# Sparse attention with two MLP layers: the context of 384 queries in one visit instead of two

## The reference

```python
scores = scale * np.matmul(q, k.transpose(0, 1, 3, 2))
thresh = np.max(scores, axis=-1, keepdims=True) - tau
scores = np.where(scores >= thresh, scores, -1e9)
scores = scores - np.max(scores, axis=-1, keepdims=True)
attn = np.exp(scores)
attn = attn / (np.sum(attn, axis=-1, keepdims=True) + 1e-9)
x = np.matmul(attn, v)                    # then to (2304, 512)
h = np.maximum(x @ w_in, 0.0)             # (2304, 2048)
x = (s * h * h + b) @ w_out               # first layer, (2304, 512)
h = x @ w_in2
y = (h / (1.0 + np.exp(-1.702 * h))) @ w_out2
```

## Time and profile before

| | us |
|---|---|
| median of 3 runs | 1021.88 |
| lowest, highest | 1020.71, 1023.87 |
| the profiled execution | 1022.94 |
| its span, first to last instruction | 1021.1 |
| PE busy | 989.9 |
| DVE busy | 801.5 |
| POOL busy | 657.9 |
| ACT busy | 605.1 |

### The profile page before, as it was taken

How to read it: one execution, slowest core, us unless ns; L and a number is a source line. 1 busy time by engine, 2 the same in 40 slices (tenths; PEclk the granted TensorE clock), 3 DMA queues, 4 the chain that set the end, 5 groups by cost and what they waited for, 6 DMA issues and landing times.

```text
span 1021.1 us, 18040 instructions
## 1 busy us (share of the span) xinstructions
PE 989.9 (97%) x5832; PEld 890.1 (87%) x5832; DVE 801.5 (78%) x1755; ACT 605.1 (59%) x1112; POOL 657.9 (64%) x714
## 2 busy tenths in 40 slices
PE   5978999999999999999999999999999999999998
PEld 4867888888888888888899999898988989889897
DVE  5999999999999999999646766877667777556563
ACT  5876665666676667665545755654546545454453
POOL 5758997778888788887657775444544544445442
PEclk9999999999999999999999999999999999999999
DMA  6228777688877887768733540112123121231212
GB/s 194 89 77 228 219 203 221 173 242 226 211 208 186 236 209 214 206 177 215 205 122 125 184 148 32 39 66 83 42 83 123 63 83 43 82 132 55 83 47 78
DMA packets 101420, 144.26 MB, mean 141 GB/s; under 512 B 10704, under 2 KB 72784, under 8 KB 101328
## 3 DMA queue, kind: packets, MB, share of 16 engines
q1 hardware_dynamic: 101328, 143.11, 48.5%
HBM read 102.96 MB, written 4.72 MB: 105 GB/s over the span
## 4 chain that ended last, share of the span: by engine, by line
PE 82%; DVE 12%; issue 2%; DMA 2%; ACT 1%; POOL 1%; SPq 0%; DVEq 0%; ACTq 0%; POOLq 0%
PE shared L810 12%; PE y_ps L829 11%; PE y_ps L927 9%; PE shared L903 9%; PE scores L927 9%; PE scores L729 7%; PE scores L903 7%; PE scores L786 6%; PE scores L810 5%; PE y_ps L849 4%; DVE scores L1010 4%; DVE prob L1036 3%; DVE blocks L1050 2%; PE scores L849 1%; DMA a_raw<-twin_in 1%
## 5 line engine op out<-in xcount | busy, mean ns | idle before, releaser
L1229 ACT ACTIVATE prob<-scores,neg_max 128x576 f32<-128x576 f32 (+1 forms) x160 | 118.9, 743 | 132.2 <-DVE scores L1010 130.0
L1568 POOL TENSOR_TENSOR a_sum_lo<-a_sum,a_hi 128x256 fp32r<-128x256 f32 x96 | 70.0, 740 | 187.4 <-DVE scores L1132 124.6
L1517 POOL TENSOR_TENSOR w_lo<-w_raw,win_hi 128x512 fp32r<-128x512 f32 x96 | 129.0, 1344 | 23.0 <-ACT win_hi L1267 18.7
L1010 DVE TENSOR_SCALAR_CACHE_REDUCE scores<-scores,consts 128x576 f32<-128x576 f32 (+1 forms) x160 | 129.3, 808 | 16.3 <-PE scores L729 14.8
L1524 POOL TENSOR_TENSOR w_lo<-w_raw,wout_hi 128x512 fp32r<-128x512 f32 x96 | 125.7, 1310 | 23.2 <-ACT wout_hi L1274 23.2
L1511 POOL TENSOR_SCALAR prob<-prob,row_inv 128x576 f32<-128x576 f32 (+1 forms) x160 | 126.1, 800 | 12.0 <-DVE row_inv L1024 11.7
L1036 DVE SCALAR_TENSOR_TENSOR prob<-scores,limit,prob 128x576 f32<-128x576 f32 (+1 forms) x160 | 128.3, 809 | 0.8 <-DVE limit L1017 0.5
L810 PE MATMUL shared<-act_hi,win_hi 128*128 128x384 f32 x280 | 95.3, 340 | 5.4 <-DVE gate L1066 3.4
L1050 DVE STREAM_TRANSPOSE blocks<-prob 128x576 f32<-128x576 f32 (+1 forms) x136 | 97.2, 752 | 3.1 <-DMA prob_t<-blocks 2.8
L810 PE MATMUL shared<-act_hi,w_lo 128*128 128x384 f32 x280 | 95.0, 339 | 0.0
L810 PE MATMUL shared<-act_lo,win_hi 128*128 128x384 f32 x280 | 94.5, 338 | 0.0
(11 more groups left out here) (154 smaller groups left out, 2934.3 us busy)
## 6 DMA issues: line engine op xcount, KB each, us to landing
w_raw<-slabs SPq DMA_DIRECT2D x93, 512.0 KB, 4.2
a_raw<-twin_in SPq DMA_DIRECT2D x24, 512.0 KB, 4.6
o_raw<-twin_out SPq DMA_DIRECT2D x24, 512.0 KB, 3.6
prob_t<-blocks SPq DMA_DIRECT2D x96, 120.0 KB, 2.8
k_raw<-k SPq DMA_DIRECT2D x32, 288.0 KB, 4.5
prob_t<-blocks SPq DMA_DIRECT2D x96, 96.0 KB, 2.8
v_sb<-v SPq DMA_DIRECT2D x26, 320.0 KB, 4.3
q_raw<-q SPq DMA_DIRECT2D x40, 192.0 KB, 4.5
```

Of the source, the lines that this page charges most:

```text
L1010: nc.vector.tensor_scalar(place, place, scale_c[0:m, :], None, ALU.mult, ALU.min, accum_out=neg_max[0:m, j % STATS:j % STATS + 1]).then_in ...
L1229: nc.scalar.activation(prob[0:m, j % PROBS, :].rearrange("p (a n) -> p a n", a=2), scores[j % 2][0:m, :, 0:HALF], ACT.Exp, bias=neg_max[0: ...
L1517: nc.gpsimd.tensor_tensor(in_of(w_lo, n), in_of(w_raw, n), win_hi[n % IN_HI][:].bitcast(F32), ALU.subtract).then_inc(win_lo_ready, 1)
```

## The change

The two pieces of a long group become one of 384 queries. It rides on one beat, 7 behind the group's first (6 for w = 29, which HASTY now names as well as w = 11): 10 matmuls into columns 288 to 479 of the first bank of the second tile's buffer, a wait for quads 2 and 3, and 10 matmuls into the same columns of the second bank. ScalarE and VectorE each take 384 columns in one instruction. The moves into either half of `prob_t` now wait for the whole piece of a long group, and a short group behind a long one has all three quads in the beat four behind its first. Long groups from w = 12 on are 12, so 40 riding pieces become 28. Short groups keep their pieces' places.

```diff
-HASTY = 3 * PAIRS_PER_BATCH - 1
+HASTY = (3 * PAIRS_PER_BATCH - 1, len(GROUPS_OF) - 3)
...
-        after = 3 if w < PE_GROUPS else 5 if w == HASTY else 6
-        pieces += [(w, n, FIRST_BEAT[w] + after + n) for n in range(3 if w < PE_GROUPS else 2 if is_long(w) else 1)]
+        if w < PE_GROUPS:
+            pieces += [(w, n, FIRST_BEAT[w] + 3 + n) for n in range(TILES_PER_HEAD[LONG])]
+        else:
+            pieces.append((w, 0, FIRST_BEAT[w] + (7 if is_long(w) else 6) - (1 if w in HASTY else 0)))
...
-    return PIECE if rides(piece) else P
+    return GROUPS_OF[PIECES[piece][0]][3] if rides(piece) else P
...
-                   if n < w and (n % 2 == 0 if n < PE_GROUPS else (place if is_long(n) else half_of(n)) == half))
+                   if n < w and (n % 2 == 0 if n < PE_GROUPS else is_long(n) or half_of(n) == half))
...
-            return scores[1][:, 1, HALF:HALF + PIECE] if rides(piece) else shared[:, 0:P]
+            if not rides(piece):
+                return shared[:, 0:P]
+            return scores[1][:, 0 if is_long(PIECES[piece][0]) else 1:2, HALF:HALF + SHORT]
...
-                    if beat == FIRST_BEAT[w] + (4 if is_long(w) else 3) + a // 2:
+                    if beat == FIRST_BEAT[w] + (4 + a // 2 if is_long(w) else 4 if is_long(w - 1) else 3 + a // 2):
                         move_quad(w, a)
...
+                for n in range(piece_size(piece) // SHORT):
+                    quads = (2 * n, 2 * n + 1) if is_long(w) else (0, 1, 2)
+                    for a in quads:
+                        half = moved_into(w, a)
+                        pe.wait_ge(moved[half][a], 64 * moves_before(w + 1, half, a))
+                    start = LONG * (n if is_long(w) else half_of(w))
+                    for c in range(KEY_CHUNKS):
+                        for side in range(2):
+                            place = piece_bank(piece)[64 * side:64 * side + 64, n, :]
...
+                            mm = nc.tensor.matmul(place.rearrange("p (a q) -> p a q", a=len(quads)),
+                                                  v_sb[:, i % 2, side, c, :], rows,
+                                                  start=(c == 0), stop=(c == KEY_CHUNKS - 1))
                 mm.then_inc(context_ready, 1)
...
-                nc.vector.tensor_tensor(act_at(act_lo, c, start, piece_size(piece)), piece_bank(piece),
-                                        act_at(act_hi, c, start, piece_size(piece)).bitcast(F32),
+                nc.vector.tensor_tensor(piece_of(act_lo, piece), piece_bank(piece), piece_of(act_hi, piece).bitcast(F32),
...
-                nc.scalar.copy(act_at(act_hi, c, start, piece_size(piece)), piece_bank(piece)
-                               ).then_inc(context_hi_ready, 1)
+                nc.scalar.copy(piece_of(act_hi, piece), piece_bank(piece)).then_inc(context_hi_ready, 1)
```

More of the change, by code:

```diff
@@ L34 @@
 LONG, SHORT = 384, 192
-PIECE = SHORT
 TILES_PER_HEAD = {LONG: 3, SHORT: 2}
@@ L290, in pieces_on @@
 def pieces_on(w, half):
-    return 1 + max(piece for piece, (n, place, _) in enumerate(PIECES)
-                   if n < w and (n % 2 == 0 if n < PE_GROUPS else (place if is_long(n) else half_of(n)) == half))
+    return 1 + max(piece for piece, (n, _, _) in enumerate(PIECES)
+                   if n < w and (n % 2 == 0 if n < PE_GROUPS else is_long(n) or half_of(n) == half))
 def value_loads():
@@ L595, in piece_bank, with piece_of @@
         def piece_bank(piece):
-            return scores[1][:, 1, HALF:HALF + PIECE] if rides(piece) else shared[:, 0:P]
+            if not rides(piece):
+                return shared[:, 0:P]
+            return scores[1][:, 0 if is_long(PIECES[piece][0]) else 1:2, HALF:HALF + SHORT]
+        def piece_of(parts, piece):
+            c, start = piece_place(piece)
+            place = act_at(parts, c, start, piece_size(piece))
+            return place.rearrange("p (n q) -> p n q", q=SHORT) if rides(piece) else place
         block = ctx.enter_context(nc.Block())
@@ L761, in context_of @@
                 w, n, _ = PIECES[piece]
[L762 to L767, removed]
+                i = VALUE_OF[piece]
+                pe.wait_ge(v_loaded[i % 2], 16 * (i // 2 + 1))
+                if not rides(piece):
                     pe.wait_ge(tail_copied, FIRST_BEAT[w] + n + 1)
@@ L772, in context_of @@
                         pe.wait_ge(context_lo_ready, piece)
[L773 to L779, removed]
+                    for c in range(KEY_CHUNKS):
+                        for side in range(2):
+                            start = LONG * side + P * n
+                            mm = nc.tensor.matmul(piece_bank(piece)[64 * side:64 * side + 64, :],
+                                                  v_sb[:, i % 2, side, c, :], turned_rows(w)[:, c, start:start + P],
+                                                  start=(c == 0), stop=(c == KEY_CHUNKS - 1))
@@ new lines, in context_of @@
+                    mm.then_inc(context_ready, 1)
+                    return
+                for n in range(piece_size(piece) // SHORT):
[4 more added lines that the diff above has]
+                    start = LONG * (n if is_long(w) else half_of(w))
+                    for c in range(KEY_CHUNKS):
+                        for side in range(2):
+                            place = piece_bank(piece)[64 * side:64 * side + 64, n, :]
@@ L1054, in context_lo @@
             def context_lo(piece):
-                c, start = piece_place(piece)
                 dve.wait_ge(context_hi_ready, piece + 1)
-                nc.vector.tensor_tensor(act_at(act_lo, c, start, piece_size(piece)), piece_bank(piece),
-                                        act_at(act_hi, c, start, piece_size(piece)).bitcast(F32),
+                nc.vector.tensor_tensor(piece_of(act_lo, piece), piece_bank(piece), piece_of(act_hi, piece).bitcast(F32),
                                         ALU.subtract).then_inc(context_lo_ready, 1)
@@ L1233, in context_hi @@
             def context_hi(piece):
-                c, start = piece_place(piece)
                 act_eng.wait_ge(context_ready, piece + 1)
-                if start >= HALF_TOKENS and piece_place(piece - 1)[1] < HALF_TOKENS:
+                if piece_place(piece)[1] >= HALF_TOKENS and piece_place(piece - 1)[1] < HALF_TOKENS:
                     act_eng.wait_ge(scores_ready, key_tiles(2 * HEADS_PER_BATCH - 1)[-1] + 1)
-                nc.scalar.copy(act_at(act_hi, c, start, piece_size(piece)), piece_bank(piece)
-                               ).then_inc(context_hi_ready, 1)
+                nc.scalar.copy(piece_of(act_hi, piece), piece_bank(piece)).then_inc(context_hi_ready, 1)
             def copy_main(j):
```

## The result

| us | before | after |
|---|---|---|
| median, beside each other, 6 runs each | 1022.31 | 1027.76 |
| lowest, highest | 1020.71, 1023.87 | 1026.94, 1029.59 |
| the profiled execution | 1022.94 | 1027.94 |
| its span | 1021.1 | 1026.2 |

The ratio is 1.0057 (95%: 1.0046 to 1.0068): slower by 5.5 us, more than the 0.3% that can be told from no change. The forecast was 1027.1 us.

What follows compares the result with a forecast made beforehand. TensorE and VectorE were both taken as nearly full, the order of light and heavy beats deciding which waits. +2.9 and +2.4 made +5.3 us on the profiled 1022.94, 1028.2; as median 1027.1, range 1019.5 to 1033.5.

Steps and rivals of the forecast that it cites:

- The order of beats, +2.9: Beats 31 to 77: two beats without a visit in a row cost VectorE more than TensorE needs; +2.9 us, bounds -2.0 and +5.
- The single spans: Visit start to visit start: 24.3 us over three N (beats without a visit), 20.14 per three-beat period, 32.6 per five-beat period.
- The 0.77 us of a beat with context: VectorE's wait for the second tile's scores before row_max in a beat with a visit, time it cannot save up.
- The moves of w = 29, +2.4: Beat 79: quads 2 and 3 land late, TensorE stops 2.1 us mid-visit (bounds 0 and 5); +2.4 us in all.
- the moves elsewhere, costed at nothing: Other groups' moves start later but stay hidden, in long groups but for half a microsecond at worst; no cost.
- rival 4: Transfers late everywhere: each of eleven long groups behind a double visit loses 0.5 us; 1033 us, chance 0.12.
- The visit itself: A double visit takes TensorE 2 x 1.77 = 3.54 us; 12 changes of 0.17 us fall away, 2.0 us off TensorE.
- VectorE's idle time ahead of the second row_max: Sign: in each double-visit beat this idle time grows to over 2 us.
- The idle times in front of double visits: Sign: TensorE waits 0.3 to 0.8 us for VectorE's mask in front of each double visit.
- Rival 1: Fewer, wider instructions win: 1018.3 us, chance 0.07; test: beat 38's visit starts under 15.9 us after beat 35's ends.

Runs made afterwards that it cites:

- e3: The changed kernel with all four quads' 16 moves of a long group in one row, ahead of the loads between: 1024.96 us, 1.0027 of the kernel before.
- the light row_max: row_max on the first 288 keys alone, in three kernels: before 1012.81 us, after 1013.38, after with the 16 moves in one row 1009.11.
- e1: The changed kernel, but w = 29 keeps its two visits in beats 79 and 80: 1025.62 us, 1.0030 of the kernel before.
- e2: The kernel before with the double visit for w = 29 alone: 1023.20 us, 1.0012 of the kernel before.
- g2: e3 with row_max on the first 288 keys alone: 1009.11 us, 0.9866 of the kernel before.
- b: The kernel before with row_max on the first 288 keys alone: 1012.81 us, 0.9916 of the kernel before.
- e4: The kernel before, its visits and moves kept, but 384-column copies behind a long group's second visit (not w = 29): 1023.36 us, 1.0012 of before.
- f2: e3 with gated_lo ahead of the second row_max in every beat with a visit: 1024.67 us, 1.0031 of the kernel before.
- f1: The kernel before with gated_lo ahead of the second row_max in every beat with a visit: 1024.11 us, 1.0022 of the kernel before.
- g1: e3 with gated_lo ahead of the second row_max in double-visit beats alone: 1023.05 us, 1.0004 of the kernel before.
- g4: g1 with the first tile's mask also ahead of the second row_max in double-visit beats: 1024.63 us, 1.0022 of the kernel before.
- a: The changed kernel with row_max on the first 288 keys alone: 1013.38 us, 0.9923 of the kernel before.

## Why the prediction was right

- **The order of beats, +2.9.** Right, and shown by itself in e3: 301.33 us from beat 31 to 77 against 301.3, without a late move. That VectorE causes it is shown by the light row_max: without late moves in front of the double visits merging costs 2.6 us with the full one and gains 3.1 with the light one. The single spans in e3 came out near what was worked out: 24.3 for three N, 19.8 to 20.7 for periods of three beats (20.14 forecast), 32.6 to 32.9 for those of five (32.6). That the sum agrees to 0.1 us is in part chance: the visits were 0.14 us shorter than in the forecast and the spans between them about as much longer. The 0.77 us of a beat with context was read from one beat; before, such waits were 0.2 to 0.8 us long.
- **The moves of w = 29, +2.4.** The gap was 2.44 us against 2.1. From beat 77's visit to beat 84's it is 43.97 us against 39.83, 4.14 longer; the forecast's share was 2.4 and 1.77 for the longer last visit, 4.17. By e1 the shares were 2.5 and 1.63. Its cause was told too simply: in e2, where the group before is not merged, the gap is 0.83 us. That nothing behind it takes the time back was said from the earlier trace rows, which end at 494.64; it held, with 507.6 us from beat 84's visit to the end of the span before and 507.8 after.
- **The term that was mis-sized: the moves elsewhere, costed at nothing.** "Hidden too, but for half a microsecond at worst" held for the gap (0.54 us in beat 38, and a smaller one in beat 57), not for what follows: from 31 to 77 the kernel after took 302.69 us against e3's 301.33, so 1.4 us, a part of rival 4. In it are the two gaps and the waits of transposes for `blocks`, 3.8 us of VectorE's time after and none in e3, which were not tried apart. I had taken its bound from one landing of 5.8 us; after, landings of 6.8 and 7.6 us stood behind four loads.
- **What made up for it.** By these spans the kernel should be 2.51 + 4.14 = 6.65 us slower. Beat 31's visit came 1.78 us earlier in the profiled execution, for which see the last section, and so the profiled executions are 5.0 us apart where the forecast had 5.3. That is luck. How much of it is in the medians, which lie 5.5 us apart, is not known, since the starts of the other runs are not; their interval, 4.7 to 7.0 us, holds both the forecast and the 6.65.
- **The visit itself.** Forecast 3.54 us, measured 3.40: for the twelve, 1.7 us less of TensorE's time than I had. That the changes to and fro fell away shows in g2 against b, where TensorE decides; in the kernel after nothing of either is gained.
- **Not as foretold.** VectorE's idle time ahead of the second row_max did not grow to over 2 us in each double visit: up to beat 77 it was 0.4 to 2.1 us and in one of them nothing, with 1.3 to 1.4 the usual, and only in beat 79, with its stop, 4.2. A VectorE that comes late has less to wait. The idle times in front of double visits were 0.16 to 0.67 us where 0.3 to 0.8 stood; a part of the lateness shows at `hidden`, which waits for `gated` (1.3 us in seven waits).

Rival 1's test, the visit of beat 38 within 15.9 us of the end of that of 35, fails: 216.09 - (196.06 + 3.40) = 16.63. The rule behind it (the Trainium skill, Perfetto Trace Analysis, Optimizing Scalar/DVE Operations) on wider operations is borne out in their total and not in the time: from 31 to 84 VectorE's 313.32 us became 311.73, and the kernel slower. The section's other sentence, that breaking up instructions may let work complete sooner, is for an engine that is not saturated but causes bubbles on others. VectorE was busy 92% of 31 to 84 before, so it may not be meant for this case; e4 points the way that it says.

## What to carry to other kernels

When two engines are both about 95% busy or more (here TensorE and VectorE up to beat 77) and tied by a buffer in each step, look at which steps are heavy for which. Gathering the heavy steps of one makes long runs of light ones, in which the other sets the pace; here what it saved in total fell into waits. Before merging two uses of a buffer, ask what was refilled between them: here half a buffer's moves lost a visit of lead, and loads among them made it a stop. An instruction moved into idle time helps only until the next wait behind it, so name that wait first.

## What the runs showed of the hardware

**The start.** Timelines of PE, the scores of the first beats, before and then after:

```profile
21.67 0.85 PE L729 MATMUL scores<-k_hi,q_hl 128*128 128x288 f32 x2 [0.89 <-DVE prob L1036]
```
```profile
21.28 0.53 PE L738 MATMUL scores<-k_hi,q_hl 128*128 128x288 f32 x2 [0.89 <-DVE prob L1049]
```

Before, these matmuls still took the longer duration at 21.67 us and the shorter one, 0.53, at 26.98; after, they were short at 21.28. e2, e3 and f2 were like before, as were b and g2; e1, e4, f1, g1, g4 and a were like after. Of the kernels with the same work ahead of beat 31, the first have its visit at 173.44 to 173.53 and the others at 171.55 to 172.40. The granted clock reads 1.00 in both stretches, so no row names the cause. 1.0 to 2.0 us of a profiled execution hang on it, and two executions are to be compared from a point behind it. How the runs that were only timed fell is not known.

**One instruction, several durations.** The same VectorE instruction (`gated_lo`, 128x384) took 0.60 us at 131.18 and 0.92 at 261.21 in f1. Its mean from 172 to 476 us was 684 ns before and 755 in f1, so it became longer when it was moved in the beat. What it runs beside and whether that is the cause was not tried.

**Landings.** The same move of 32 rows lands 2.2 to 2.4 us after its issue when no load stands ahead of it (those issued at 199.62 to 204.18 in the kernel after), and 4.5 to 7.6 behind four loads. In e3, where the loads stand behind all sixteen, the same group's moves land within 2.2 to 3.2 us.
